# Gated scan, token mixing and two channel MLPs on one core: tile 5's x taken from the accumulator bank, and channel weights loaded in another order

## What is computed

```python
# 1. gated complex scan: q, k, v, a_re, a_im are (4, 8, 768, 48)
mag = np.sqrt(a_re * a_re + a_im * a_im)
scale = np.minimum(mag, 0.999) / (mag + 1e-06)
for t in range(S):                       # state (4, 8, 48, 48), complex
    new_re = ar * S_re - ai * S_im
    new_im = ar * S_im + ai * S_re
    kv = np.einsum('bhd,bhe->bhde', k[:, :, t], v[:, :, t])
    S_re, S_im = (new_re + kv, new_im)
    y[:, :, t] = np.einsum('bhd,bhde->bhe', q[:, :, t], S_re)
# x = y as (4, 768, 384)
# 2. mixer
h = np.maximum(xt @ w_tok1, 0.0) @ w_tok2      # over the sequence, d_tok 256
u = x + h.transpose(0, 2, 1)
x = u + np.maximum(u @ w_ch1, 0.0) @ w_ch2     # over the channels, d_ch 1536
# 3. layer norm and a second channel MLP
xn = (x - mu) / np.sqrt(var + 1e-06) * g_ln
out = x + np.maximum(xn @ w2_ch1, 0.0) @ w2_ch2
```

## Time and profile before

| | before |
|---|---|
| executions, us | 860.89, 861.41, 857.54 |
| median, us | 860.89 |
| profiled execution, us | 861.4 |
| its span, us | 859.6 |
| TensorE busy, matmuls / weight loads | 815.5 us (95%) / 796.2 us (93%) |
| VectorE / ScalarE busy | 473.2 us (55%) / 419.1 us (49%) |
| chain that ended last | 54% TensorE, 1% transfers, 1% VectorE |

### The profile page before, as it was taken

One profiled execution on the slowest core, in us unless ns is written; L12 is line 12 of the kernel. 1 busy time (PEld: TensorE's weight loads), 2 busy tenths in 40 slices (PEclk: granted clock), 3 DMA queues, 4 the chain that ended last, 5 costly groups with the idle time before them and its releaser, 6 DMA issues.

```text
span 859.6 us, 16499 instructions
## 1 busy us (share of the span) xinstructions
PE 815.5 (95%) x6902; PEld 796.2 (93%) x6902; DVE 473.2 (55%) x811; ACT 419.1 (49%) x758; POOL 26.5 (3%) x39
## 2 busy tenths in 40 slices
PE   0498899999999999999999999999999999999998
PEld 0397899999999999999999999999999999999998
DVE  6997888786777777666834633443133223312122
ACT  7988788778387777477732512222112111211111
POOL 1011000010001000000000000000000000000000
PEclk9999999999999999999999999999999999999999
DMA  9899754565525654443426200000020002000000
GB/s 359 223 161 198 193 131 84 100 130 113 102 47 101 123 121 111 78 86 70 93 38 227 76 1 1 1 1 28 1 83 1 29 9 75 28 1 28 1 28 29
DMA packets 46701, 71.16 MB, mean 83 GB/s; under 512 B 5024, under 2 KB 38048, under 8 KB 46112
## 3 DMA queue, kind: packets, MB, share of 16 engines
q1 hardware_dynamic: 46624, 70.09, 34.8%
HBM read 42.86 MB, written 8.26 MB: 59 GB/s over the span
## 4 chain that ended last, share of the span: by engine, by line
PE 54%; DMA 1%; DVE 1%; SPq 0%; issue 0%; ACT 0%
PE bank L378 17%; PE bank L380 17%; PE bank L379 17%; PE bank L1760 1%; PE bank L1665 1%; DMA rows<-hats 1%; PE bank L1683 0%; PE bank L1687 0%; PE bank L1653 0%; SPq L537 0%; PE bank L1700 0%; DVE turned_x L1388 0%; PE bank L1813 0%; DVE hats L1234 0%; DVE qk_t L1221 0%
## 5 line engine op out<-in xcount | busy, mean ns | idle before, releaser
L844 ACT ACTIVATE hidden<-bank 128x384 fp32r<-128x384 f32 x192 | 94.1, 490 | 345.2 <-PE bank L380 345.2
L1309 DVE SCALAR_TENSOR_TENSOR hidden<-bank,hidden 128x384 fp32r<-128x384 f32 x192 | 106.2, 553 | 255.0 <-ACT hidden L844 255.0
L378 PE MATMUL bank<-ch,hidden 128*128 128x384 f32 x576 | 192.7, 335 | 0.1
L380 PE MATMUL bank<-ch,hidden 128*128 128x384 f32 x576 | 192.7, 335 | 0.0
L379 PE MATMUL bank<-ch,hidden 128*128 128x384 f32 x576 | 192.4, 334 | 0.0
L378 PEld LDWEIGHTS bank<-ch,hidden 128*128 128x128 f32 x576 | 108.1, 188 | 0.9 <-DVE hidden L1309 0.5
L379 PEld LDWEIGHTS bank<-ch,hidden 128*128 128x128 f32 x576 | 108.1, 188 | 0.0
L380 PEld LDWEIGHTS bank<-ch,hidden 128*128 128x128 f32 x576 | 108.1, 188 | 0.0
L378 PE MATMUL bank<-turned_x,ch 128*128 128x384 f32 x288 | 102.3, 355 | 0.3 <-DVE hidden L1309 0.3
L380 PE MATMUL bank<-turned_x,ch 128*128 128x384 f32 x288 | 96.9, 336 | 0.0
L379 PE MATMUL bank<-turned_x,ch 128*128 128x384 f32 x288 | 96.7, 336 | 0.0
(11 more groups left out here) (175 smaller groups left out, 1433.6 us busy)
## 6 DMA issues: line engine op xcount, KB each, us to landing
rows<-hats SPq DMA_DIRECT2D x120, 128.5 KB, 4.7
a_t<-in_a_rows_dram SPq DMA_DIRECT2D x18, 384.0 KB, 5.3
qk_t<-in_qk_rows_dram SPq DMA_DIRECT2D x18, 384.0 KB, 5.8
v_t<-in_v_cols_dram SPq DMA_DIRECT2D x24, 192.0 KB, 5.5
plain_ch<-in_moe_w_ch_dram SPq DMA_DIRECT2D x6, 768.0 KB, 8.4
out_dram<-x_u SPq DMA_DIRECT2D x24, 192.0 KB, 1.9
x_kept_dram<-x_u SPq DMA_DIRECT2D x18, 192.0 KB, 3.1
x_u<-x_kept_dram SPq DMA_DIRECT2D x18, 192.0 KB, 3.2
```

Source lines behind the costliest of these rows:

```text
L378: nc.tensor.matmul(ps, lhs_h, rhs_h, start=first, stop=False, skip_group_check=True)
L380: return nc.tensor.matmul(ps, lhs_l, rhs_h, start=False, stop=final, skip_group_check=True)
L844: nc.scalar.activation(hid_h[:, m % NHID, :], hid_ps[m % 2][:, 0:HALF], ACT.Relu).then_inc(hidden_rounded, 1)
L1309: nc.vector.scalar_tensor_tensor(out=hid_l[:, m % NHID, :], in0=hid_ps[m % 2][:, 0:HALF], scalar=0.0, in1=hid_h[:, m % NHID, :].bitcast(F3 ...
```

## The change

Tile 5's x goes another way. ScalarE rounds straight from the bank into `xs_h` (`round_y`), VectorE makes the remainder straight from the bank (`rest_y`), and the copy into x (`keep_y`) comes after VectorE's remainder and after `angle(4)`. TensorE runs three fillers (FILL_X = 3) ahead of tile 5's mix-down, and the six matmuls stand in another order: the four that need only `xs_h` first, then the two that need `xs_l`. Five fillers (FILL_H = 5) instead of four follow; mix-up starts with half 0 for tiles 0 and 1, waiting for that half only, then half 1 for the same tiles, then a wait for `x_kept`, then tiles 2 to 5 as before.

SyncE's list changes: v of tile 5 is loaded ahead of piece 2; pieces 3 and 4 no longer follow piece 2; piece 3 stands where piece 6 stood, behind piece 5; both halves of rows 7 come ahead of v of tile 7, then piece 6, v of tile 8, piece 4, piece 7. The order in which the pieces are split is unchanged. A fallback path (`slow`) keeps the old way.

```diff
             load_qk(3)
+            load_v(5)
             load_piece(2)
-            load_piece(3)
-            load_v(5)
-            load_piece(4)
             load_a(5)
             lay_rows(6, 0)
             lay_rows(6, 1)
             wait_rows(sp, NT - 1)
             load_piece(5)
-            load_piece(6)
+            load_piece(3)
             load_a(6)
             load_v(6)
             load_qk(4)
             lay_rows(7, 0)
+            lay_rows(7, 1)
             load_v(7)
-            lay_rows(7, 1)
+            load_piece(6)
             load_v(8)
+            load_piece(4)
             load_piece(7)
             load_qk(5)
...
+            def round_y(n):
+                act.wait_ge(outputs_ready, 2 * n + 2)
+                nc.scalar.activation(xs_h[:, n % NT, :], y_ps[:, 0:C], ACT.Copy).then_inc(x_rounded, 1)
+
+            def keep_y(n):
+                b, j = divmod(n, NT)
+                act.wait_ge(x_split, splits_through(n))
+                nc.scalar.activation(x_tile(b, j), y_ps[:, 0:C], ACT.Copy).then_inc(x_kept, 1)
...
                 round_piece(act, 2)
-                keep_x(5, slow)
-                round_x(5)
+                if slow:
+                    keep_x(5, slow)
+                    round_x(5)
+                else:
+                    round_y(5)
                 angle(4)
+                if not slow:
+                    keep_y(5)
                 round_tok_hidden(0, 0)
...
+            def rest_y(n):
+                dve.wait_ge(x_rounded, splits_through(n))
+                nc.vector.tensor_tensor(xs_l[:, n % NT, :], y_ps[:, 0:C], xs_h[:, n % NT, :].bitcast(F32), ALU.subtract).then_inc(x_split, 1)
...
                 log_scan(4)
-                rest_x(5)
+                if slow:
+                    rest_x(5)
+                else:
+                    rest_y(5)
                 half_turn(4)
...
+            def mix_down_last():
+                j = NT - 1
+                ws = [[t[:, j, rt * P:(rt + 1) * P] for t in (tok1_h, tok1_l)] for rt in range(RT)]
+                pe.wait_ge(x_rounded, NT)
+                for rt in range(RT):
+                    for w in ws[rt]:
+                        nc.tensor.matmul(r1_ps(0)[rt][:, 0:C], w, xs_h[:, j, :], start=False, stop=False, skip_group_check=True)
+                pe.wait_ge(x_split, NT)
+                for rt in range(RT):
+                    nc.tensor.matmul(r1_ps(0)[rt][:, 0:C], ws[rt][0], xs_l[:, j, :], start=False, stop=True, skip_group_check=True).then_inc(tok1_done, 1)
...
-                for rt in range(RT):
-                    for j in mix_order(b) if b else (NT - 1,):
-                        mix_down(b, rt, j)
+                if b:
+                    for rt in range(RT):
+                        for j in mix_order(b):
+                            mix_down(b, rt, j)
+                else:
+                    for i in range(FILL_X):
+                        keep_busy()
+                    mix_down_last()
...
-                    for i in range(4):
+                    for i in range(FILL_H):
                         keep_busy()
-                    pe.wait_ge(tok_hidden_split, RT)
-                    for j in range(NT):
+                    for rt in range(RT):
+                        pe.wait_ge(tok_hidden_split, rt + 1)
+                        for j in range(2):
+                            mix_up(b, rt, j)
+                    pe.wait_ge(x_kept, NT)
+                    for j in range(2, NT):
                         for rt in range(RT):
                             mix_up(b, rt, j)
```

More of the change, by code:

```diff
@@ L51, in gated_scan_mixer_mlp_kernel @@
     MAG_CAP = 0.999
+    FILL_X = 3
+    FILL_H = 5
     MAG_EPS = 1e-6
@@ L1420, in keep_flag, with rest @@
                 nc.vector.tensor_copy(flag[:, :], flag_ps).then_inc(flag_set, 1)
-            def rest():
+            def rest(slow):
                 add_state(0)
@@ L1633, in _ @@
             with dve.If(flagged < 1):
-                rest()
+                rest(False)
             with dve.Else():
                 slow_dve(dve)
-                rest()
+                rest(True)
         @block.tensor
```

## The result

| | before | after |
|---|---|---|
| executions | 20 | 20 |
| median, us | 858.01 | 859.44 |
| lowest to highest, us | 855.81 to 861.41 | 858.30 to 861.65 |
| profiled execution, us | 861.4 | 859.2 |

The ratio after to before is 1.0025, with a 95% interval of 1.0015 to 1.0035: slower by 2.1 us (1.3 to 3.0), within the 0.5% that the prediction took for no change. The range 857.5 to 866.5 held the time. The number 862.5 is 3 us too high, because it was built on a profiled execution of 861.4, while the kernel before has its median at 858.0 over 20 executions; the reason for that is a finding of its own.

What follows compares the result with a forecast made beforehand. TensorE was taken to bound the kernel, passing early gains and losses to the end. From the profiled 861.4 us: minus 2.0 (x path), 0 (early loads), plus 3.1 (late loads) gave 862.5, range 857.5 to 866.5.

Steps and rivals of the forecast that it cites:

- What bounds the kernel: TensorE, nearly always busy from 200 us on: what it gains or loses before about 120 us reaches the end unchanged.
- Edit 1: Tile 5's x rounded straight from the bank: mix-up starts at 94.95 in place of 96.99, minus 2.0 us.
- Edit 2: Early loads, pieces 3 and 4 moved later, v of tile 5 ahead of piece 2: tile 4's 2.54 us stall stays, 0.
- All engines waited there: At tile 4's stall, 81.88 us: reason given for its 2.5 us passing on to the end if it goes.
- Edit 3: Late loads: piece 6 behind rows 7 makes ScalarE's rounding 6.9 us late, and TensorE loses 3.1 us.
- Slack 1.84: Tile 7's chunk state at 134.19 waits for the second k copy, ended 132.35: 1.84 us set against ScalarE's 4.9 us lateness.
- slower rival: Piece 6 lands 8.4 us after issue, 2.8 us more, and half clock near 124 and 134 adds 1.5: 866.8; chance 0.13.
- The stall goes: The stall at 81.88 us in tile 4 vanishes with the emptier data queue, 2.5 us gained: 860.0; chance 0.25.
- Piece 6's wait costs nothing: ScalarE catches up after its late rounding before TensorE needs it: 859.4; chance 0.12, two thirds with the stall gone.
- The bank path saves nothing: At tile 5's x, another step turns up between and no time is saved: 864.5; chance 0.08.

Runs made afterwards that it cites:

- edit 1 alone: Kernel before with only tile 5's x from the bank, its fillers and matmul order, old load order kept: 855.52 against 857.04 us, ratio 0.9984.
- the version with piece 4 late: Kernel before plus the new x path, v of tile 5 ahead of piece 2, rows 7 ahead of v of tile 7, only piece 4 moved behind them: 0.9981.
- the two runs at full clock: Kernel before with the changed load order and old x path, ratio 1.0044; kernel before with only piece 6 moved behind both halves of rows 7, 1.0037.
- 38 fillers: New x path with the old load order, 38 fillers instead of 34 ahead of the first tile: one execution, 863.05 us.
- the run without fillers: New x path with the old load order and FILL_X = 0: one profile, 3.45 us from tile 5's last output to mix-up.

## Why the prediction was right or wrong

**What bounds the kernel: right.** The difference between the two traces is -2.4 us at tile 8 and -2.2 at the end; what was won or lost before 139 us reached the end nearly whole.

**Edit 1: right in kind, near in size.** Forecast -2.0; at mix-up the traces show -1.8 in the changed kernel, -2.2 with edit 1 alone, and the time -1.4 (0.9984). The order of the last steps was as worked out: rounding, remainder, scan, hidden remainder. The difference of 0.4 between the two traces goes with the stall (3.44 to 3.45 us to mix-up in all five profiles of the new path with it, 3.82 to 3.85 in the three without). In the changed kernel's first profile, without it, VectorE was still at work on unit 4 when the rounding ended (87.26 + 0.49 = 87.75) and began `rest_y` only at 88.19, without idle time. With edit 1 alone it had stood idle for 0.72 us and began as soon as the rounding was done:

```profile
91.74 0.56 DVE L1283 TENSOR_TENSOR turned_x<-bank,turned_x 128x384 fp32r<-128x384 f32 x1 [0.72 <-ACT turned_x L834]
```

What is late next, once TensorE comes earlier, is VectorE's own list. The forecast had worked from a profile with the stall. By the times most executions have none, and the new path without a stall is the 1.6 us one; that would make the gain in the time the smaller one, but it is not shown.

**Edit 2: the zero was right in the time, the reading behind it was not.** The forecast put the stall down to a late instruction fetch, which the moved place bears out. It then took the stall as a fixed part of the kernel before. For the changed kernel it is a part of some executions, and for the kernel before the two groups of times say the same. The changed kernel's first profile lacks it, its second has 2.0 us, with the same loads. My argument from the data in front of the fetch did not foresee that. And "All engines waited there" is too strong: from 82 to 85 us ScalarE was busy for 1.80 of the 3 us. In the time, the version with piece 4 late (0.9981) and edit 1 with the full early queue (0.9984) are the same, so thinning the early queue has no worth in the time that these runs can tell.

**Edit 3: right in mechanism, wrong in the last place, 0.5 us too small.** Forecast: piece 6 lands 5.6 us after issue (5.7), ScalarE waits 6.9 us (7.06), TensorE first waits about 1.5 at the up-projection (1.60), loss 3.1. Measured loss: 3.6. The step that failed is the place of the last wait and with it "Slack 1.84": the prediction set ScalarE's 4.9 us of lateness against the slack of the second k copy at tile 7's chunk state. ScalarE was late by that much (the copy came 4.86 us later than before, counted from tile 7's first k turn), but TensorE was stopped earlier in its list, before the second half of tile 7's scores. What it waited for there was VectorE's first mask, which stands behind the hidden remainder 4; it was 5.1 us late with 1.6 us of slack. At the chunk state nothing was left to wait for: the second k copy ended at 130.76 + 0.48 = 131.24, and TensorE reached it at 131.80. The prediction followed the lateness down ScalarE's list and did not follow it through VectorE's. That the second wait has the size forecast for it (1.52 and 1.50 us in the two runs at full clock, "about 1.5") is luck. The half clock, which the prediction had in the slower rival at 1.5 us on top, came in the changed kernel and cost nothing, since it ran beside that wait.

**The sum.** In differences the forecast was +1.1 (3.1 - 2.0), the result +2.1 (1.3 to 3.0). Of the missing 1.0, 0.5 is the mask's smaller slack in edit 3, and the rest lies inside the interval and the spread of edit 1 (-1.4 in time for -2.0). The step that failed for the number 862.5 is the first term, 861.4: a profiled execution that held a 2.5 us stall, beside a median of three of which two lay above 860. Over 20 executions the median is 858.0, so this term was 3.4 us too high, the largest error in the sum. The prediction saw the stall and named it, and still used that execution as the base without asking how many of the others had it.

**The rivals.** "The stall goes": seen in one of two profiles, no difference between versions in the time. "Piece 6's wait costs nothing": false, 21.67 against 18.09 us. "Slower, with a long landing and the half clock": the landing was the short one, the half clock came and cost nothing. "The bank path saves nothing": false in the traces, and likely false in the time.

## What to carry to other kernels

When a load is moved back in a queue, find the instruction that consumes it and the whole list queued behind that instruction: here a transfer that TensorE did not need yet cost it 3.6 us, because one rounding stood at its old place, and nothing once the rounding was moved as well. Before a profile serves as the base of a sum, look whether its stalls recur: a stall of 2.5 us that is in some executions only is larger than most edits of this kind. And when a lateness is priced, follow it through every engine's list and take the smallest slack on the way: here the nearest place was two engines on, in VectorE's mask. A stretch at half clock behind such a wait costs only what is not already covered by the lateness; here that was nothing.

## What was not expected of the hardware

- TensorE stood for 1.4 to 2.5 us at one place of its instruction list, in a run of small matmuls, in nine of twelve profiles. The place moved with the instruction count, and the instruction packet came 3 us and more later than in the profiles without a stall. Whether it happened went with a start that differed by about 1 us (42.00 and earlier against 42.55 and later). Why the start differs, and why that decides, stays open.
- The length of a wait of TensorE didn't tell whether the clock fell. The stall of 2.54 us left it full, one of 2.28 us (38 fillers) was followed by the 0.50 level. Waits of 1.64 and 1.67 us before the up-projection left it full, waits of 1.60 and 1.61 us at the same place were followed by the 0.50 level, and so was the old path's wait of 1.83 us in all four profiles. A wait of 0.68 us in the run without fillers left it full.
